# Row sums of query tiles 2 to 4 corrected and inverted together in a fused attention and MLP kernel

## The reference

```python
scores = scale * q @ k.T + bias            # window of 128 keys, causal, slope per head
attn = exp(scores - max(scores))
attn = attn / (sum(attn) + 1e-09)
x = attn @ v                               # heads side by side: (4, 576, 512)
ch = relu(layernorm(x) * g_ln @ w_ch1) @ w_ch2       # 512 -> 2048 -> 512
y = x + ch
h = relu(y @ w_in)                         # 512 -> 1024
out = (h * sigmoid(conv3(h))) @ w_out
```

## Time and profile before

| | |
|---|---|
| median of 3 runs | 835.75 us (835.41 to 836.39) |
| profiled execution, first to last instruction (span) | 834.8 us |
| PE busy | 786.3 us (94%) |
| DVE busy | 547.0 us (66%) |
| ACT busy | 385.0 us (46%) |
| POOL busy | 171.7 us (21%) |

### The profile page before, as it was taken

One profiled execution on the slowest core, in us unless ns is written; L12 is line 12 of the kernel. 1 busy time (PEld: TensorE's weight loads), 2 busy tenths in 40 slices (PEclk: granted clock), 3 DMA queues, 4 the chain that ended last, 5 costly groups with the idle time before them and its releaser, 6 DMA issues.

```text
span 834.8 us, 17035 instructions
## 1 busy us (share of the span) xinstructions
PE 786.3 (94%) x5792; PEld 765.4 (92%) x5792; DVE 547.0 (66%) x1510; ACT 385.0 (46%) x1063; POOL 171.7 (21%) x155
## 2 busy tenths in 40 slices
PE   4776788999999999999999999999999999999998
PEld 3665778999999999998999999999998999999998
DVE  4997677777367777645677754522229887788862
ACT  5775456565224655512556632122235444444442
POOL 4553675211011211101112200021120110111100
PEclk9676799999999999999999999999999999999999
DMA  5441554221122123013121201411312122221101
GB/s 154 106 130 48 156 162 127 60 78 43 58 65 66 38 71 101 8 58 102 29 71 51 86 8 61 134 58 54 89 49 76 31 79 78 78 78 47 59 22 44
DMA packets 64425, 60.81 MB, mean 73 GB/s; under 512 B 23904, under 2 KB 52576, under 8 KB 63840
## 3 DMA queue, kind: packets, MB, share of 16 engines
q1 hardware_dynamic: 64352, 59.87, 24.3%
HBM read 45.69 MB, written 14.16 MB: 72 GB/s over the span
## 4 chain that ended last, share of the span: by engine, by line
PE 69%; DVE 11%; issue 11%; POOL 3%; ACT 2%; DMA 2%; SPq 1%; POOLq 0%; DVEq 0%; ACTq 0%
PE bank L1009 20%; PE bank L1011 19%; PE bank L1010 19%; PE bank L950 4%; PE bank L964 3%; PE bank L980 3%; DVE prob L741 2%; DVE q_st L829 1%; DMA w_stage<-w 1%; DMA q_raw<-qT 1%; DVE ch_stage L741 1%; POOL rstd L482 1%; DVE rows L734 1%; ACT prob L562 1%; DVE rows L736 1%
## 5 line engine op out<-in xcount | busy, mean ns | idle before, releaser
L1009 PE MATMUL bank<-h_hi,wb_hi 128*128 128x288 f32 x512 | 156.9, 306 | 3.1 <-DVE h_lo L798 2.3
L1009 PE MATMUL bank<-xn_hi,wa_hi 128*128 128x288 f32 x512 | 157.0, 307 | 2.7 <-issue 1.4
L1010 PE MATMUL bank<-xn_lo,wa_hi 128*128 128x288 f32 x512 | 152.0, 297 | 0.0
L1011 PE MATMUL bank<-xn_hi,wa_lo 128*128 128x288 f32 x512 | 152.0, 297 | 0.0
L1011 PE MATMUL bank<-h_hi,wb_lo 128*128 128x288 f32 x512 | 151.6, 296 | 0.0
L1010 PE MATMUL bank<-h_lo,wb_hi 128*128 128x288 f32 x512 | 151.5, 296 | 0.0
L798 DVE SCALAR_TENSOR_TENSOR h_lo<-bank,h_hi 128x288 fp32r<-128x288 f32 x128 | 58.1, 454 | 109.8 <-ACT h_hi L594 108.5
L594 ACT ACTIVATE h_hi<-bank 128x288 fp32r<-128x288 f32 x128 | 52.3, 409 | 164.1 <-PE bank L1011 163.1
L1009 PEld LDWEIGHTS bank<-h_hi,wb_hi 128*128 128x128 f32 x512 | 97.1, 190 | 5.2 <-issue 3.9
L1009 PEld LDWEIGHTS bank<-xn_hi,wa_hi 128*128 128x128 f32 x512 | 97.6, 191 | 4.0 <-issue 3.2
L1010 PEld LDWEIGHTS bank<-xn_lo,wa_hi 128*128 128x128 f32 x512 | 97.7, 191 | 0.0
(11 more groups left out here) (95 smaller groups left out, 1752.0 us busy)
## 6 DMA issues: line engine op xcount, KB each, us to landing
k_raw<-kT SPq DMA_DIRECT2D x64, 144.0 KB, 2.8
q_raw<-qT SPq DMA_DIRECT2D x64, 144.0 KB, 2.9
w_stage<-w SPq DMA_DIRECT2D x32, 256.0 KB, 3.0
x_in<-x_spill SPq DMA_DIRECT2D x8, 580.0 KB, 4.3
ch_in<-ch_spill SPq DMA_DIRECT2D x8, 580.0 KB, 5.2
x_spill<-xT SPq DMA_DIRECT2D x4, 1152.0 KB, 5.3
ch_spill<-ch_stage SPq DMA_DIRECT2D x32, 144.0 KB, 1.9
out<-out_stage SPq DMA_DIRECT2D x32, 144.0 KB, 1.8
```

What stands on the lines that cost most here:

```text
L1009: nc.tensor.matmul(dst, w_h, a_h, start=start, stop=False)
L1010: nc.tensor.matmul(dst, w_h, a_l, start=False, stop=False)
L1011: last = nc.tensor.matmul(dst, w_l, a_h, start=False, stop=stop)
```

## The change

Group B is no longer normalised by itself. The call for group C corrects and inverts the row sums of tiles 2, 3 and 4 with one instruction each on 128 rows, after the exponential of tile 4, and then multiplies all three tiles. Tile 4 has only 64 rows, so the other half of its column is set by a memset of `rows3` at the start, with the waits that this needs. The queues of the other engines keep their order.

```diff
@@ gpsimd
+            nc.gpsimd.memset(rows3[:], 1.0).then_inc(zeros_ready, 1)
             nc.gpsimd.memset(v_raw[:, 4, :], 0.0).then_inc(zeros_ready, 1)
@@ sync
-            sp.wait_ge(zeros_ready, 1)
+            sp.wait_ge(zeros_ready, 2)
@@ vector
             def normalise(batch, h, x):
+                if x == "B":
+                    return
                 hd = H * batch + h
-                t0, t1 = GROUP[x][0], GROUP[x][-1] + 1
+                t0, t1 = (0, 2) if x == "A" else (2, NT)
                 rows = TILES[t0][0]
-                step = 2 * (3 * hd + "ABC".index(x))
+                step = 2 * (2 * hd + "AC".index(x))
                 dve.wait_ge(exp_ready, NT * hd + t1)
@@ vector
+            dve.wait_ge(zeros_ready, 1)
             run("prologue", 0)
@@ tensor
-            pe.wait_ge(zeros_ready, 5)
+            pe.wait_ge(zeros_ready, 6)
```

## The result

The changed kernel takes 862.46 us (median of 4 runs, 860.98 to 864.5) against 835.62 us (4 runs); the ratio is 1.0315, 95% interval 1.0287 to 1.0343. The direction and the mechanism are those of the prediction, the time lies inside its range (847 to 865), but 7.5 us above the predicted 855.0. The profiled execution took 860.98 us with a span of 859.2: 24.4 us more than before, where the working had 19.1.

What follows compares the result with a forecast made beforehand. PE bounds the stretch with MLP (296.4 of 300 us busy), DVE the heads of batch 0. 19.5 - 0.7 + 0 + 0.3 = 19.1 us on the 834.8 span gives 853.9, with the surplus 855.0; range 847 to 865.

Steps and rivals of the forecast that it cites:

- The price of one head: Later batches: PE waits at PT A for tile 2's multiply, 0 to 1.33 us per head; third batch 7.5 us.
- a late PE only moves the chain along: `q_lo` hangs on PE's own scores through k_lo and ACT's copies, so PE cannot catch up and each head pays anew.
- the pair: Group C's correction and reciprocal on DVE, widened to three columns on 128 rows: 0.40 us, ends 0.36 and 0.45.
- heads 2 to 7 of the second batch: PE's waits at PT A in these heads: 1.30 + 0.85 + 0.18 + 0.61 + 1.40 + 0 = 4.3 us.
- Heads 0 and 1 of the second batch: Weight-splitting stage: 1 to 2 us more wait at head 0's PT A against an earlier xT; 0, ends -2 and +3.
- Batch 0: Heads without MLP, bound by DVE: some multiplies later, some pairs saved; sum +0.3 us, ends -1 and +1.5.
- the two waits for xT that went: From 200 to 500 us, PE's two waits for xT vanish because its work is done in time: -0.7 us.
- The clock: Rival: waits at PT A drop PE to half clock; about 5 large waits +7 us, all +22; 861 to 880, chance 0.13.
- Absorbed: Rival: min C, `q_lo` and copies come earlier, each wait shrinks by half: 845 us; 838 to 849, chance 0.12.
- gain: Rival: tile 2's multiply still precedes PT A everywhere; batch 0 saves 2.5 us, giving 833.2; chance 0.02.
- nothing: Rival: the two effects cancel, which needs the same early multiply of tile 2: 835.7 us, chance 0.03.
- The surplus over the span: Median of the runs lies 0.95 us above the span; the same was added to 853.9, giving 854.9, say 855.0.

Runs made afterwards that it cites:

- tile 2 back: The changed kernel, but tile 2 is corrected, inverted and multiplied alone in group B's place, tiles 3 and 4 together in group C's: 849.2 us, ratio 1.015.
- C ahead of `q_lo`: The changed kernel, but outside batch 0 DVE normalises group C before `q_lo` instead of behind it: 856.66 us, ratio 1.0239.
- transposes later: The changed kernel, but PT A and PT B stand further back in PE's own order: 862.69 us, ratio 1.0315.

## Why the prediction was right, and where its size was off

**The price of one head: right.** Third batch 7.60 against 7.54, head by head within 0.5. The forecast that a late PE only moves the chain along, so that each head pays anew, holds: from head 0 to head 7 a head takes 13.25 us on average instead of 12.12, and a plain one (heads 0 and 1) 12.9 instead of 11.7, where the prediction said 13.1 instead of 11.8. That the sum fits to 0.06 us is in part luck, since errors in single heads nearly cancel: in heads 2 and 3 of the third batch 1.67 instead of 1.31 and 0.87 instead of 0.95, in head 4 0.63 instead of 0.17, in head 5 0.91 instead of 1.28. Head 2's excess is the widened correction: priced at 0.40 for the pair with 0.45 as the upper end, it took 0.71 + 0.18 there because it, too, waits for v_lo. Head 4's excess is v_lo as well: the prediction counted it in heads 1, 2, 5 and 6 only, but here it runs from 326.99 to 327.86 and holds the multiply of 327.13, and PT A follows at 328.06. For the stretch of heads 2 to 7 of the second batch 4.3 was forecast and 5.57 measured, up to the third batch.

**Heads 0 and 1 of the second batch: the term that was mis-sized.** I took 0, with +3 as the upper end; the stretch from batch 0's end to head 2 grew by 3.34. Leaving these heads as before gives 4.7 us back by the medians, 3.6 by the spans (855.6 and 859.2), 2.7 of it at head 2. Two parts of the working came true. In head 0 PT A comes 8.10 us after the scores of tile 4 instead of 6.97, so 1.13 later, where 1 to 2 were forecast; the wait of 3.50 stands partly in the place of one for h_lo shortly before, which was 2.35 us before the change and is 1.15 now. And the wait for xT fell from 1.68 to 0.24 us. What the sum had at nothing is PT A of head 1: PE waits 3.74 us there and PT A comes 7.32 us after the scores instead of 5.66, since the prediction left correction and multiplies at their old length beside a POOL that works almost without a gap. They took 1.12 and 2.19 us. The gain at xT is used up by that. Of the 3.34 us, 1.13 and 1.66 lie at the two PT A; the rest was not placed.

**The queue behind: not in the sum.** The prediction named PT A and the products after it as what is queued behind. DVE's own queue behind the moved multiplies (xT, `pt_lo`, h_lo and with it `ch_stage`) it left out. In the changed kernel that is small, since PE is late too: `ch_stage` 1.9 us instead of 0.7. But it decides what a repair is worth. Three experiments that took most or all of the wait at PT A away (tile 2 back, C ahead of `q_lo`, transposes later) got 13, 6 and 0 of 26 us back, and tile 3's multiply alone, which PT A never waits for, costs 6. PE was busy 296 of 300 us, so DVE's 105 idle microseconds there were no margin; the margin was how early each single result came, over 2 us for tile 2 and nothing for xT, for which PE already waited twice.

**Batch 0: sign not settled, weight nil.** +0.3 was forecast; the trace of the change has -0.83, the one with only batch 0 changed -0.36. Eight of the kernels here run the change's instructions in that stage, and its end lies between 67.47 and 69.52 in their traces, against 69.52 in the one trace of the kernel before. So such a figure moves by up to 2 us from one execution to another; a small gain is likely, but with one trace of the kernel before it is not shown. In the time no gain is left at the end. The pace of a head there, 8.4 us (10.00 to 68.69 over seven), is as forecast, and so are the 64 corrections instead of 96 and the two waits for xT that went (0.7 us forecast).

**The clock: the rival did not come.** Behind the waits at PT A of 1.59 us and less PE stayed at 2.4 GHz, as behind the one of 1.64 before; 3.50 and 3.74 were each followed by a stretch at 1.2 GHz. The changed kernel has as many such stretches behind batch 0 as the one before, two in the profiled execution. The rival's premise, that a wait a little longer would cost the clock, was met by 1.68 before and three times with later transposes (1.90, 1.90, 1.89). But the length of the wait does not decide alone: with only batch 0 changed PE waited 2.47 us (to 119.58) and 2.45 us (to 136.57), with heads 0 and 1 as before 1.90 and 2.32, and the granted clock stayed 1.00 from 100 to 160 us in both.

**Absorbed, gain, nothing: refuted.** No head's wait was halved; tile 2's multiply came after `q_lo` in every head that has one ahead of it. That a gain needs tile 2 ahead of PT A was only half of the condition: the version that had it (tiles 0 to 3 in group B's place) is still 0.2% slower.

**The surplus over the span.** The sum added 0.95 us to the span, and 0.1 by rounding. But the 0.95 compared the span of the profiled execution with the median of others: in every execution on record, of either kernel, the time lies about 1.8 us above its own span. In the changed kernel the profiled execution also has the shortest span of the four (859.2 to 862.7). Together the median lies 3.3 us above the profiled span instead of 1.1, and that is the other 2.2 us of the 7.5, beside 5.3 on the span.

## What to carry to other kernels

Where the bound engine is full, what counts on the other engines is by how much each result comes early, not their idle time. Before two instructions are merged, list the readers of every result that waits for the last of them, and also what stands behind the merged group in its own queue: that second list cost as much here as the first once the first was repaired. Two small instructions saved per head on an engine with a third of its time idle were worth nothing, and one 0.35-us multiply delayed past its reader cost 0.6 to 1.7 us in each of seven heads of a batch. A moved operation must be priced at its new place, beside what other engines run there.

## What the runs showed of the hardware

In these traces the width of a tiny DVE operation decides whether POOL holds it up. In the middle of POOL's v_lo the correction of the row sums took 0.15 us on 64x1 before (at 290.08, v_lo from 289.73 to 290.79) and 0.28 for three of 128x1. On 128x3 it took 0.71 and 0.72 and ended with v_lo (301.28 against 301.26, 294.67 against 294.64); with no POOL instruction beside it 0.16 to 0.17. Two columns are held up as well: in the kernel before a correction on 128x2 took 0.91 us and ended with POOL's wb_lo (115.85 against 115.83). The reciprocal of three columns, in v_lo's middle as well (301.54 above), took its usual 0.17: the kind of operation matters too. The Trainium skill (Advanced Engine Details and Errata, "VectorE Performance Modes") states the condition of the mode that uses the port shared with GpSimd: source and destination in SBUF, and their non-unit major dimensions both even, or both odd, above one and equal. A single column has no such dimension, three columns have; the durations agree. The prediction used the lock for the multiplies and overlooked that the correction comes under it when it gets more than one column.
